# Column loads one step ahead, the u product on GpSimd, and the bonus sum ahead of the mask in a chunked linear-attention kernel

## The chip, the cores and the metric

The kernel runs on one core of one Trainium2 chip. The metric is the device time of one execution in microseconds. Three runs of the kernel before gave 383.59, 384.34 and 384.41 us, a median of 384.34 us. One further execution was profiled; it took 385.27 us, and its trace spans 383.5 us from the first instruction to the last.

## The reference

Three stages follow one another: a gated linear attention with a bonus term, a soft mixture of experts (MoE), and a feed-forward layer.

```python
# attention: B, H, S, D = 4, 8, 768, 48
for t in range(S):
    kt, vt, rt = (k[:, :, t], v[:, :, t], r[:, :, t])
    cur = np.einsum('bhd,bhe->bhde', u[None] * kt, vt)
    y[:, :, t] = np.einsum('bhd,bhde->bhe', rt, state + cur)
    state = w[None, :, :, None] * state + np.einsum('bhd,bhe->bhde', kt, vt)
# soft MoE: logits = x @ phi; softmax over tokens, 8 experts (384 x 1024 x 384) on 4 slots each,
# softmax over slots to combine
# feed-forward: h = x @ w_in; g = h * sigmoid(1.702 * h); out = g @ w_out      (384 -> 2048 -> 384)
```

## The kernel before

The attention is computed in 6 chunks of 128 tokens. A chunk has one **step** for each of the 4 batches, so there are 24 steps; this text numbers them n = 4 * chunk + batch, and calls them step 0 to step 23. Chunk 0 and chunk 5 are written out; chunks 1 to 4 are one loop body of four steps that each engine runs four times.

For each step three tensors are loaded by the SP queue: `rk` (r and k with channels on partitions, "the columns", 512 KB), `kr` (k and r with tokens on partitions, "the tokens", 384 KB) and `v` (192 KB). `rk` and `kr` are double buffered. The SP queue is in order: a load whose buffer is not free holds up every load behind it. `load_rk(n)` (L262) waits until VectorE has scaled step n - 2; `load_kr(n)` (L271) waits until GpSimd has made the scaled keys `kk` of step n - 2; behind them come `v` and a piece of the expert weights `w1` (L284).

What the engines do for step n:

- VectorE, `scale(n)` (L766): two tensor_tensor, columns times powers of w, out of a table in PSUM, into `rks`. It waits for the columns and for `rs_used`, which TensorE counts up at `earlier`.
- GpSimd, `bonus(n)` (L1199): the product k * r into `rkn`, and, from chunk 1 on, a second one, `rkn` times u (`ubc`, u on all partitions). In chunk 0 that second product is VectorE's (L782). Then `scaled_keys(n)` (L1211), then `bonus_values(n)` (L1219): v times the bonus sums, into `vd`.
- VectorE, `bonus_sum(n)` (L775): one reduction of `rkn` over the channels into `dds`; `bonus_values(n)` waits for it.
- TensorE, `scores` (L370), which waits for both masks of the step before and for `rks`; VectorE, `mask(n)` (L788): two copy_predicated that move the scores that count from PSUM to `at`.
- TensorE, in the order of its step n (L481): `logits` of the chunk before (batch 1 only), `earlier(n - 1)` (the old state's part of the output), `scores(n)`, in chunk 0 only `bonus_turns(n - 1)`, then `outputs(n - 1)`, `state(n - 1)`, small transposes (`turns` in batch 1), `tokens(n - 2)`, and from step 3 on `bonus_turns(n)`, which transposes `vd` of the same step and waits for it (`vd_ok`, L394); `gather` in batch 2.
- ScalarE: `decay` multiplies the state by w^128 (four small activations), `columns` and `rows` move results out of PSUM. `new_state(n)` (L803) on VectorE adds the chunk's part to the state.

VectorE's order inside step n before (L846): `slot_max` of the last chunk (batch 1), then `scale(n + 1)`, `mask(n)` (in steps 1 to 3 the other way round), `bonus_sum(n + 1)`, `running` of the last chunk (batch 3), `new_state(n - 1)`. The bonus sum of a step is thus taken in the step in front of it.

In chunk 5, GpSimd has extra work: after `bonus_values(21)` it makes the `own` tiles (L1245), after `bonus_values(22)` a subtraction over 128x640, and before `bonus_values(23)` a product over 128x640 (L1240), whose factor comes from VectorE's `row_sum` and that one from ScalarE's exponential of the subtraction. TensorE waits for that product (`c_ok`) in step 23.

After step 23 the MoE (to about 157 us) and the feed-forward (to the end) follow, on TensorE nearly without a gap.

Of the kernel before, what the change touches and what calls it, by code (L numbers as in the profile page):

```python
# [12 lines left out]
P = 128  # L13
# [29 lines left out]
WARM = 10  # L43
# [8 lines left out]
def rwkv_soft_moe_ffn(nc, rk, kr, v, wcol, u, phi, w1, w2, win, wout, ident, strict, match, jsel, sel, parts, out):  # L52
    with ExitStack() as ctx:
# [10 lines left out]
        def sem(name):  # L64
# [127 lines left out]
            sem(n) for n in ("lt_ps", "l_ok", "cm_ok", "nm_ok", "ex_ok", "al_ok", "tr_ps", "tr_ok", "p_ps", "run_ok"))  # L192
        nm_new, l_new, mask_go, tiles_go = (sem(n) for n in ("nm_new", "l_new", "mask_go", "tiles_go"))
# [65 lines left out]
        def _(sp):  # L259
# [28 lines left out]
            def step(c, b, first, count):  # L288
                load_rk(c, b)
                load_kr(c, b)  # L290
                load_v(c, b)
                load_w1(first, count)
# [3 lines left out]
            load_kr(0, 0)  # L296
            load_rk(0, 1)
            load_v(0, 0)
            load_kr(0, 1)
            load_v(0, 1)  # L300
            step(0, 2, 0, 0)
# [57 lines left out]
        def _(pe):  # L359
# [10 lines left out]
            def scores(c, b):  # L370
# [11 lines left out]
                if is_first(c, b):  # L382
# [4 lines left out]
                    keep_warm(LG, 7)  # L387
# [331 lines left out]
        def _(dve):  # L719
# [55 lines left out]
            def bonus_sum(c, b):  # L775
                n = B * c + b
                if is_first(c):

                    dve.wait_ge(rk_ok, n + 1)
                    if b == 0:  # L780
                        dve.wait_ge(s_const, 16 * 2)
                    dve.tensor_tensor(rkn[:, b % 2, :, :], rkn[:, b % 2, :, :], ubc[:, :, :], ALU.mult)\  # L782
                       .then_inc(rku_ok, 1)
# [4 lines left out]
            def mask(c, b):  # L788
                n = B * c + b
                if is_first(c, b):  # L790
                    dve.wait_ge(zeroed, 5)
                    dve.wait_ge(s_const, 16 * 2)
# [10 lines left out]
            def new_state(c, b):  # L803
                n = B * c + b
                dve.wait_ge(st_ps, n + 1)
                dve.wait_ge(sdec, HP * (n + 1))
# [39 lines left out]
            def step(c, b):  # L846
# [4 lines left out]
                if is_first(c) and b:  # L851
                    mask(c, b)
                    scale(*following(c, b))
                else:
                    if more:
                        scale(*following(c, b))
                    mask(c, b)
                if is_last(c) and b == 2:
                    row_sum(*early)
                if more:  # L860
                    bonus_sum(*following(c, b))
# [132 lines left out]
        def _(act):  # L994
            act.dma_start(idt[:, :], ident).then_inc(s_ident, 16)
            for dst, src in ((ubc[:, :, :].rearrange("p h e -> p (h e)"), u.partition_broadcast(P)),
                             (keep[:, :], strict)):
                act.dma_start(dst, src).then_inc(s_const, 16)
# [58 lines left out]
            def step(c, b):  # L1057
# [5 lines left out]
                if not is_first(c, b):  # L1063
                    if not is_last(prev(c, b)[0]):
# [126 lines left out]
        def _(pool):  # L1191
# [7 lines left out]
            def bonus(c, b):  # L1199
# [6 lines left out]
                if is_first(c):  # L1206
                    return
                pool.wait_ge(rk_ok, n + 1)
                pool.tensor_tensor(rkn[:, s, :, :], rkn[:, s, :, :], ubc[:, :, :], ALU.mult).then_inc(rku_ok, 1)
# [117 lines left out]
```

## Time and profile before

| | us |
|---|---|
| median of three runs | 384.34 |
| profiled execution, its own time | 385.27 |
| its span (first to last instruction) | 383.5 |
| TensorE busy in the span | 369.9 (96%) |
| VectorE / ScalarE / GpSimd busy | 235.0 / 189.4 / 94.5 |
| chunk 0 and start, up to the first TensorE instruction of chunk 1's first step | 0 to 26.1 |
| chunks 1 to 5 | 26.1 to about 119 |
| granted TensorE clock | 1.000 throughout |

Times in the trace are microseconds from the start of the span. A merged row (xN) covers N instructions that follow one another. GpSimd is POOL, VectorE is DVE, ScalarE is ACT, TensorE is PE in the rows. The bracket at a row's end says how long the engine sat idle before it and what ended the wait. The start of a matmul row is when it begins; the next one begins before the modelled end of the one before.

### The profile page before, as it was taken

The numbers are of one execution on the slowest core, as the hardware profiler recorded it, in microseconds if no ns is written. First come the engines' busy times: TensorE is split into PE (matmuls) and PEld (weight loads), VectorE is DVE, ScalarE is ACT, GpSimd is POOL, SyncE is SP. The second block draws the span as 40 slices with busy tenths as digits, with TensorE's granted clock in tenths as the row PEclk, the third lists the DMA queues.
The fourth block names the chain that finished last, engine by engine and source line by source line (L and its number), as shares of the span: only waits on it lengthen the run. The fifth ranks groups of instructions, "written<-read, shape, count | busy, mean of one in ns | idle before, by whom it ended". The sixth has DMA issues, their size and how long they took to land.

```text
span 383.5 us, 9099 instructions
## 1 busy us (share of the span) xinstructions
PE 369.9 (96%) x3206; PEld 290.6 (76%) x3206; DVE 235.0 (61%) x433; ACT 189.4 (49%) x409; POOL 94.5 (25%) x110
## 2 busy tenths in 40 slices
PE   5698999999999999999999999999999999999996
PEld 5677788878777344577888888888888888888885
DVE  6978787878774301587756556555555555555550
ACT  1344554545434440676564456445644564465452
POOL 4678788878682020100000000000000000000000
PEclk9999999999999999999999999999999999999999
DMA  7899999999999999600011002000200020002002
GB/s 234 286 333 344 400 393 405 399 393 354 405 327 409 390 414 413 249 0 2 1 46 38 0 0 84 0 0 0 82 0 0 0 82 0 0 0 82 0 2 82
DMA packets 21797, 63.76 MB, mean 166 GB/s; under 512 B 3088, under 2 KB 6816, under 8 KB 21392
## 3 DMA queue, kind: packets, MB, share of 16 engines
q1 hardware_dynamic: 20864, 63.09, 43.4%
q10 hardware_dynamic: 912, 0.39, 0.5%
q8 instruction: 14, 0.23, 0.2%
q14 instruction: 7, 0.06, 0.0%
HBM read 58.75 MB, written 4.72 MB: 165 GB/s over the span
## 4 chain that ended last, share of the span: by engine, by line
PE 92%; DVE 2%; DMA 2%; issue 1%; ACT 1%; POOL 1%; SPq 0%; DVEq 0%; ACTq 0%
PE bank L638 11%; PE bank L637 11%; PE bank L636 11%; PE bank L378 6%; PE pair L426 6%; PE pair L636 6%; PE pair L637 6%; PE pair L638 6%; PE bank L623 4%; PE pair L414 3%; PE pair L397 3%; PE bank L585 3%; PE bank L447 3%; PE bank L565 2%; DMA vb<-v 2%; PE bank L438 2%
## 5 line engine op out<-in xcount | busy, mean ns | idle before, releaser
L926 DVE TENSOR_TENSOR gf<-bank,sg 128x512 f32<-128x512 f32 x72 | 49.8, 691 | 58.3 <-ACT sg L1133 58.0
L1133 ACT ACTIVATE sg<-bank 128x512 f32<-128x512 f32 x72 | 42.9, 598 | 71.0 <-PE bank L623 71.0
L637 PE MATMUL bank<-ghi,whi 128*128 128x512 f32 x190 | 73.9, 389 | 0.0
L636 PE MATMUL bank<-glo,whi 128*128 128x512 f32 x190 | 73.9, 389 | 0.0
L638 PE MATMUL bank<-ghi,wlo 128*128 128x512 f32 x190 | 73.9, 389 | 0.0
L937 DVE TENSOR_TENSOR glo<-gf,ghi 128x512 fp32r<-128x512 f32 x96 | 66.3, 691 | 0.3
L1139 ACT ACTIVATE ghi<-gf 128x512 fp32r<-128x512 f32 x95 | 59.3, 624 | 1.8 <-DVE gf L926 1.7
L636 PEld LDWEIGHTS bank<-glo,whi 128*128 128x128 f32 x190 | 35.7, 188 | 7.4
L637 PEld LDWEIGHTS bank<-ghi,whi 128*128 128x128 f32 x190 | 35.7, 188 | 7.4
L638 PEld LDWEIGHTS bank<-ghi,wlo 128*128 128x128 f32 x190 | 35.7, 188 | 7.4
L772 DVE TENSOR_TENSOR rks<-rkb,bank 112x512 f32<-112x512 f32 x48 | 30.8, 681 | 15.4 <-PE pair L414 10.9
L636 PE MATMUL pair<-glo,whi 128*128 128x512 f32 x95 | 37.3, 392 | 0.0
L637 PE MATMUL pair<-ghi,whi 128*128 128x512 f32 x95 | 37.0, 389 | 0.0
L638 PE MATMUL pair<-ghi,wlo 128*128 128x512 f32 x95 | 37.0, 389 | 0.0
L798 DVE COPY_PREDICATED at<-keep,bank 128x512 f32<-128x512 int32 x48 | 32.5, 730 | 1.3 <-PE bank L378 0.9
L378 PE MATMUL bank<-rks 48*128 48x128 f32 x384 | 27.9, 284 | 5.2 <-DVE rks L772 3.9
L926 DVE TENSOR_TENSOR gf<-pair,sg 128x512 f32<-128x512 f32 x24 | 16.6, 692 | 23.8 <-ACT sg L1133 23.7
L378 PEld LDWEIGHTS bank<-rks 48*128 48x128 f32 x384 | 23.4, 187 | 9.5 <-issue 8.0
L1016 ACT ACTIVATE yt<-pair 112x512 f32<-112x512 f32 x24 | 14.3, 598 | 30.0 <-PE pair L426 30.0
L623 PE MATMUL bank<-ct,mst 128*128 (+1 forms) x72 | 27.9, 392 | 0.5 <-DVE mst L964 0.4
L1204 POOL TENSOR_TENSOR rkn<-krb 128x384 f32<-128x384 f32 x24 | 24.1, 1004 | 12.2 <-DMA krb<-kr 11.9
L426 PE MATMUL pair<-at,vb 128*48 128x128 f32 x384 | 25.9, 277 | 0.0
(179 smaller groups left out, 512.3 us busy)
## 6 DMA issues: line engine op xcount, KB each, us to landing
ring<-w SPq DMA_DIRECT2D x24, 512.0 KB, 6.3
rkb<-rk SPq DMA_DIRECT2D x23, 512.0 KB, 6.2
krb<-kr SPq DMA_DIRECT2D x24, 384.0 KB, 5.5
ring<-w SPq DMA_DIRECT2D x4, 1536.0 KB, 14.3
ring<-w SPq DMA_DIRECT2D x8, 768.0 KB, 8.4
vb<-v SPq DMA_DIRECT2D x24, 192.0 KB, 5.5
out<-ob SPq DMA_DIRECT2D x18, 256.0 KB, 2.1
ring<-win SPq DMA_DIRECT2D x3, 1024.0 KB, 14.3
```

The source lines that it names most:

```text
L378: last = pe.matmul(SC[i][:, hp * CH:(hp + 1) * CH], rks[s, b % 2, 1, hp, :], rks[s, b % 2, 0, hp, :], start=True, stop=True)
L426: last = pe.matmul(YT[i][o0:o0 + D, a * CH:(a + 1) * CH], vb[:, b, 2 * (a + 2 * w) + i, :], at[:, b % 2, i, a + 2 * w, :], start=False, st ...
L623: pe.matmul(HB[f % 4][:, :], mst[:, f * P:(f + 1) * P], ct_flat[:, bass.ds(i * TT, TT)], start=True, stop=True).then_inc(hh_ps, 1)
L636: pe.matmul(o, w_hi, lo, start=(f == 0), stop=False)
L637: pe.matmul(o, w_hi, hi, start=False, stop=False)
L638: pe.matmul(o, w_lo, hi, start=False, stop=(f == KF - 1)).then_inc(prod_ps, 1)
L772: dve.tensor_tensor(rks[a, b % 2, x, :, :], rkb[a, b % 2, x, :, :], w[a, :, :], ALU.mult)\
L798: dve.copy_predicated(at[:, b % 2, half, :, :], keep[:, :].unsqueeze(1).to_broadcast([P, 4, CH]), SC[half][:, :].rearrange("p (h t) -> p h ...
L926: dve.tensor_tensor(gf[:, f % 2, :], bank[f % 4][:, :], sg[:, f % 2, :], ALU.mult).then_inc(gf_ok, 1)
L937: dve.tensor_tensor(glo[:, f % 4, :], gf[:, f % 2, :], ghi[:, f % 4, :], ALU.subtract)\
L1133: act.activation(sg[:, f % 2, :], bank[f % 4][:, :], ACT.Sigmoid, scale=1.702).then_inc(sg_ok, 1)
L1139: act.activation(ghi[:, f % 4, :], gf[:, f % 2, :], ACT.Copy).then_inc(ghi_ok, 1)
```

## The change

- The SP queue asks for the columns of step n + 1 before the tokens of step n. Inside each step the order of issues is `rk(n + 1)`, `kr(n)`, `v(n)`, `w1`. The start keeps its order and asks for `rk(2)` at its end.
- u is loaded in the SP queue behind the first tokens, no more in ScalarE's queue; it has a semaphore of its own.
- In chunk 0, too, GpSimd multiplies by u.
- VectorE's step n has one order for all chunks: `scale(n + 1)`, `bonus_sum(n)`, `mask(n)`. `bonus_sum(0)` is still taken ahead of step 0.
- The decays of the state in steps 0, 1 and 2 are left out (the state is still zero there), and `new_state` waits for one less chunk of them.
- One matmul less in each of the two blocks that keep TensorE busy at the start.

```diff
-WARM = 10
+WARM = 9
@@ SP
             def step(c, b, first, count):
-                load_rk(c, b)
+                if not (is_last(c) and b == B - 1):
+                    load_rk(*following(c, b))
                 load_kr(c, b)
                 load_v(c, b)
                 load_w1(first, count)
@@
             load_rk(0, 0)
             load_kr(0, 0)
+            sp.dma_start(ubc[:, :, :].rearrange("p h e -> p (h e)"), u.partition_broadcast(P)).then_inc(s_u, 16)
             load_rk(0, 1)
             load_v(0, 0)
             load_kr(0, 1)
             load_v(0, 1)
+            load_rk(0, 2)
             step(0, 2, 0, 0)
             step(0, 3, 0, 0)
@@ TensorE, scores(0, 0)
-                    keep_warm(LG, 7)
+                    keep_warm(LG, 6)
@@ VectorE
             def bonus_sum(c, b):
                 n = B * c + b
-                if is_first(c):
-                    dve.wait_ge(rk_ok, n + 1)
-                    if b == 0:
-                        dve.wait_ge(s_const, 16 * 2)
-                    dve.tensor_tensor(rkn[:, b % 2, :, :], rkn[:, b % 2, :, :], ubc[:, :, :], ALU.mult)\
-                       .then_inc(rku_ok, 1)
                 dve.wait_ge(rku_ok, n + 1)
@@ mask
-                    dve.wait_ge(s_const, 16 * 2)
+                    dve.wait_ge(s_const, 16)
@@ new_state
-                dve.wait_ge(sdec, HP * (n + 1))
+                if is_first(c):
+                    dve.wait_ge(s_new, 1)
+                else:
+                    dve.wait_ge(sdec, HP * (n - B + 2))
@@ step
-                if is_first(c) and b:
-                    mask(c, b)
+                if more:
                     scale(*following(c, b))
-                else:
-                    if more:
-                        scale(*following(c, b))
-                    mask(c, b)
+                if not is_first(c, b):
+                    bonus_sum(c, b)
+                mask(c, b)
                 if is_last(c) and b == 2:
                     row_sum(*early)
-                if more:
-                    bonus_sum(*following(c, b))
@@ ScalarE
-            for dst, src in ((ubc[:, :, :].rearrange("p h e -> p (h e)"), u.partition_broadcast(P)),
-                             (keep[:, :], strict)):
-                act.dma_start(dst, src).then_inc(s_const, 16)
+            act.dma_start(keep[:, :], strict).then_inc(s_const, 16)
@@
-                    if not is_last(prev(c, b)[0]):
+                    if not is_first(prev(c, b)[0]) and not is_last(prev(c, b)[0]):
                         decay(*prev(c, b))
@@ GpSimd, bonus
-                if is_first(c):
-                    return
                 pool.wait_ge(rk_ok, n + 1)
+                if is_first(c, b):
+                    pool.wait_ge(s_u, 16)
                 pool.tensor_tensor(rkn[:, s, :, :], rkn[:, s, :, :], ubc[:, :, :], ALU.mult).then_inc(rku_ok, 1)
```

## Rows read from the trace of the kernel before

**Rows 1.** The page, the chain that ended last, shares of the span by engine.
```profile
PE 92%; DVE 2%; DMA 2%; issue 1%; ACT 1%; POOL 1%; SPq 0%; DVEq 0%; ACTq 0%
```
**Rows 2.** Busy time by stretch: chunk 4, all engines in turn, clock, DMA share, GB/s.
```profile
83.00:101.00 18.00, 18.00 (x329) 14.95 (x330) 14.55 (x29) 9.09 (x30) 14.08 (x15) 1.00 0.99 373
```
**Rows 3.** TensorE's timeline, steps 4 and 5: start, length, engine, line, tiles.
```profile
26.10 0.65 PE L414 MATMUL pair<-rks,st 48*48 48x128 f32 x16
...
33.05 0.42 PE L414 MATMUL pair<-rks,st 48*48 48x128 f32 x4 [1.20 <-issue]
```
**Rows 4.** VectorE's timeline in chunk 0.
```profile
9.13 0.56 DVE L782 TENSOR_TENSOR rkn<-rkn,ubc 128x384 f32<-128x384 f32 x1 [0.47 <-POOL rkn L1204]
...
13.14 1.34 DVE L782 TENSOR_TENSOR rkn<-rkn,ubc 128x384 f32<-128x384 f32 x1 [0.42 <-POOL rkn L1204]
14.51 0.55 DVE L786 TENSOR_REDUCE dds<-rkn 128x8 f32<-128x384 f32 x1
14.98 1.34 DVE L798 COPY_PREDICATED at<-keep,bank 128x512 f32<-128x512 int32 x2
```
**Rows 5.** GpSimd's timeline in chunks 0 and 1.
```profile
8.10 1.00 POOL L1204 TENSOR_TENSOR rkn<-krb 128x384 f32<-128x384 f32 x1 [3.98 <-DMA krb<-kr]
10.35 0.83 POOL L1226 TENSOR_TENSOR vd<-vb,dds 128x384 f32<-128x384 f32 x1 [1.26 <-DVE dds L786]
11.14 1.00 POOL L1216 TENSOR_TENSOR kk<-krb,wkn 128x384 f32<-128x384 f32 x1
12.10 1.00 POOL L1204 TENSOR_TENSOR rkn<-krb 128x384 f32<-128x384 f32 x1
...
24.93 1.01 POOL L1209 TENSOR_TENSOR rkn<-rkn,ubc 128x384 f32<-128x384 f32 x1
```
**Rows 6.** DMA issues and busy time by stretch, at the start.
```profile
ubc<-u ACTq DMA_DIRECT2D x1, 192.0 KB, 5.7
...
4.00:6.00 2.00, 2.00 (x12) 2.00 (x11) 1.19 (x12) 0.00 (x0) 0.12 (x1) 1.00 0.78 173
```
**Rows 7.** TensorE's timeline: end of chunk 3, start of chunk 4.
```profile
78.76 0.65 PE L414 MATMUL pair<-rks,st 48*48 48x128 f32 x16
...
82.96 0.65 PE L414 MATMUL pair<-rks,st 48*48 48x128 f32 x16
...
86.48 0.65 PE L397 MATMUL pair<-idt,vd 128*112 128x128 f32 x4
```
**Rows 8.** VectorE's timeline beside them.
```profile
79.55 1.29 DVE L772 TENSOR_TENSOR rks<-rkb,bank 112x512 f32<-112x512 f32 x2 [1.63 <-PE pair L414]
...
82.46 0.14 DVE L837 COPY stat<-stat 128x1 f32<-128x1 f32 x1
...
83.80 0.35 DVE L807 TENSOR_TENSOR st<-st,bank 112x192 f32<-112x192 f32 x1 [0.29 <-DVE acc L840]
84.39 1.28 DVE L772 TENSOR_TENSOR rks<-rkb,bank 112x512 f32<-112x512 f32 x2 [0.23 <-issue]
```
**Rows 9.** Chunk 5: TensorE's, GpSimd's and VectorE's timelines.
```profile
113.84 0.65 PE L397 MATMUL pair<-idt,vd 128*112 128x128 f32 x4 [0.17 <-ACT yt L1016]
...
118.77 0.60 PE L397 MATMUL pair<-idt,vd 128*112 128x128 f32 x4
...
106.11 0.18 POOL L1245 MEMSET own<- 128x96 f32 x1
...
107.61 1.01 POOL L1204 TENSOR_TENSOR rkn<-krb 128x384 f32<-128x384 f32 x1
...
111.16 1.26 POOL L1251 TENSOR_TENSOR lnat<-lnat,rm 128x640 f32<-128x640 f32 x1
...
107.17 1.28 DVE L772 TENSOR_TENSOR rks<-rkb,bank 112x512 f32<-112x512 f32 x2 [0.20 <-PE pair L414]
...
114.44 0.82 DVE L821 TENSOR_REDUCE rm<-lnat 128x20 f32<-128x640 f32 x1 [0.41 <-ACT lnat L1055]
```
**Rows 10.** The tile krb: from issue to landing.
```profile
DMA to landing us min/median/max: 3.2/5.5/8.4
```

More of the change, by code:

```diff
@@ L192, in rwkv_soft_moe_ffn @@
             sem(n) for n in ("lt_ps", "l_ok", "cm_ok", "nm_ok", "ex_ok", "al_ok", "tr_ps", "tr_ok", "p_ps", "run_ok"))
+        s_u = sem("s_u")
         nm_new, l_new, mask_go, tiles_go = (sem(n) for n in ("nm_new", "l_new", "mask_go", "tiles_go"))
```

## Prediction

> **What bounds the kernel now.** I read the chain of waits first, then the busy time by stretch, then the timelines of the engines side by side. The chain runs over TensorE for 92% of the span [rows 1]. In chunk 4 TensorE is busy 18.00 of 18.00 us, GpSimd 14.08, VectorE 14.55, and the DMA engines have a share of 0.99 at 373 GB/s [rows 2]. So from chunk 1 on TensorE sets the pace, and two other things stand close behind it: the DMA engines, and any result that TensorE needs just in time. Only the first 26.10 us are different. There TensorE waits again and again for VectorE and GpSimd, until `earlier(3)` opens the steps of chunk 1 at 26.10 [rows 3]. One further gap stands in step 5: 1.20 us before 33.05, which no semaphore ends ("issue") [rows 3].
>
> From this follow two rules for the sum. What is saved before 26.1 moves all that comes later forward, one for one. And from then on any wait put into TensorE's order costs its full length, as nothing behind it is idle.
>
> I write T(n) for the time at which `earlier(n - 1)` starts on TensorE in step n.
>
> **The start (a gain).** Before, VectorE multiplies by u itself: 0.56 us when GpSimd is at rest, 1.34 us beside GpSimd's product at 13.14, then the sum 0.55 and two masks 1.34 [rows 4]. After, the product by u is GpSimd's and costs 1.01 there [rows 5].
>
> The first tokens land at about 8.10 [rows 5]. u is 192 KB, took 5.7 us to land and shared the engines with the first columns and tokens, at 173 GB/s in the stretch 4:6 [rows 6]. Queued behind the tokens it no longer delays them: 192 KB are 0.5 us at the chunk rate and 1.1 us at 173 GB/s, and nothing if the rate at the start is set otherwise. I take 0.7. Then k * r of step 0 runs 7.4 to 8.4, the u product 8.5 to 9.5 (u has landed by then), the sum 9.5 to 10.05. Call its end D = 10.05 (before: 9.13 + 0.56 + 0.55, about 10.25 [rows 4]).
>
> From D on GpSimd is the chain of chunk 0. Its pitches are `vd` 0.79 (10.35 to 11.14) and 0.96 (11.14 to 12.10) for a product of 1.00 [rows 5]; the u product waits 0.1 for the one before it. One batch is therefore 0.79 + 0.96 + 0.96 + 1.06, about 3.8. The u products end at D + 3.9, D + 7.8 and D + 11.6, and each releases a sum (0.55), the masks (1.25) and the next scores. After the last one come `kk` 0.96 and `vd` 0.85, so `bonus_turns(3)` can start at D + 13.45 = 23.5. I add 0.3 for the tokens of step 2, now behind the columns of step 3 in the queue, and 0.55 for the turns themselves: T(4) = 24.3 against 26.10, a gain of **1.8**. The bounds are 0.65 (tokens no earlier, the tokens of step 2 late by 0.75) and 2.6 (tokens earlier by 1.2, no wait behind them). VectorE's masks end earlier than that chain at each batch, so they are covered.
>
> A rule of the Trainium skill speaks against this part: "GPSIMD Engine Reference", section 4.1, says to put elementwise products on VectorE, as GpSimd takes about twice the time. The rows agree on the ratio (1.01 against 0.56), but the product that ran beside GpSimd took 1.34 [rows 4], and section 8 of the same page names the reason, shared SBUF interfaces. By the rule alone the four moves would cost 4 x 0.45 = 1.8 us, and chunk 0 would gain nothing. What decides is the order, as the sum is now off the masks' way; so I do not follow it.
>
> No cost: the two dropped warm-up matmuls lie in TensorE's idle time ahead of the scores (the granted clock is 1.00 throughout [rows 2, 6]); the dropped decays lie on ScalarE, which waits most of the time; they come back nowhere, since the state is zero. The mask's u wait was long over.
>
> The 1.20 us gap in step 5 stays in my sum. It is at one place of the code, in the first pass through the loop. The Trainium skill, "Runtime: NRT & Kernel Launch", section "Instruction fetch mechanics", says instructions come in blocks by DMA; no row shows that this gap is such a fetch.
>
> **The tokens behind the columns (a small loss).** Before, `kr(n)` is asked for when `kk(n - 2)` is done. After, it stands behind `rk(n + 1)`, which waits for the scaling of step n - 1, that is until T(n - 2) + 0.79 + 1.3 [rows 7, 8]; with the issue of the columns, about T(n - 2) + 2.8. It must land by T(n) - 0.4, as k * r, times u, `kk` and `vd` (3.9 us) follow on GpSimd before TensorE wants `vd`. Two steps last 9.1 to 9.3 us, so 5.9 us are left, against a median to landing of 5.5, a least of 3.2 and a most of 8.4 [rows 10]. Hence between 0 and 2.5 us in a step. With the DMA engines full [rows 2], 512 KB more ahead of it are 1.3 us later in the queue; in chunk 0 the engines gain about that back. I take **0.3** for the whole, while the lead is largest (chunks 1 and 2).
>
> **The bonus sum one step later (the main loss).** Before, the sum of step n was taken in step n - 1, a whole step ahead of its use. After, it stands behind `scale(n + 1)`, which cannot start before T(n) + 0.79 (79.55 - 78.76) [rows 7, 8]. Then: two scalings 1.20, sum 0.55, `vd` 0.08 + 0.83, TensorE's start 0.05. So `bonus_turns(n)` can start at T(n) + 3.50. TensorE gets there at T(n) + 3.52 (86.48 - 82.96) [rows 7]. In an ordinary step the cover is just gone and costs nothing; for missed hundredths over some fifteen steps I add **0.2**, bounds 0 and 1.5 (0.1 each).
>
> In the first step of a chunk it is not enough. There VectorE comes late out of step n - 1, where it has `running` of the last chunk (82.46 on) and `new_state` (83.80): its scaling starts at 84.39, T(16) + 1.43 [rows 7, 8]. The new order of step 15 holds the same instructions, so this time stays. Then the sum starts at 85.59, ends 86.14, `vd` ends 87.05, and TensorE starts 87.1 where it started 86.48: **0.6** late. That holds for the first steps of chunks 2, 3 and 4: 1.8 us. In chunk 5, out of the loop, VectorE is quicker; I take 0.2. Bounds for one step: 0.3 (if `running` moves up) and 0.8.
>
> In chunk 5 GpSimd's extra work stands between. Before, `own` (106.11 to 107.61, 1.50 us) came with a step in hand [rows 9]. After: `scale(22)` starts at 107.17 as before [rows 9], sum of step 21 to 108.9, `vd` to 109.8, `own` to 111.3, k * r and u of step 22 (2.1) to 113.4, sum to 114.0, `vd` to 114.9; TensorE's turns of step 22 start at 114.95, before at 113.84 [rows 9]: 1.1 late. Next on GpSimd the subtraction, 1.26 [rows 9], to 116.15; ScalarE's exponential of as many columns (0.8, taken as long as VectorE's pass over them [rows 9]) and VectorE's row sum with its two small ones (1.3) give the factor at 118.3; GpSimd has made the products of step 23 by then; the product over 128x640 to 119.6, `vd(23)` to 120.45. TensorE turns it at 120.5, before at 118.77 [rows 9]: **1.7** late in all, the 1.1 included. Bounds 1.0 and 2.5.
>
> **The sum.** -1.8 + 0.3 + 0.2 + 1.8 + 0.2 + 1.7 = +2.4 us. From the end of chunk 5 on TensorE's chain passes this on. The profiled execution took 385.27 us (span 383.5 and 1.8 around it), so a like execution would take 387.7; the median of the runs lies 0.93 lower, and the forecast against it is 384.34 + 2.4 = **386.7 us**.
>
> **The rivals.**
>
> (a) *The late sum does not hold TensorE up* (faster). Place: `bonus_turns(n)` in the first steps of chunks and in chunk 5. If `vd` were there when TensorE arrives, only the start counts: 384.34 - 1.8 + 0.3 = 382.8. It decides at 0.6 us of slack per first step. For it: VectorE is busy only 14.55 of 18.00 us [rows 2], so it could run ahead. Against it: it cannot, since scaling waits for `earlier` on TensorE (idle 1.63 us for it [rows 8]). Chance 0.22.
>
> (b) *The tokens become the bound.* If the latency stays at 6.8 us, between the median and the most, against 5.9, steps lose 0.9; in four of the eight steps of chunks 1 and 2 that is 3.6 in place of 0.3: 390.0. For it: the DMA share of 0.99. Against it: loads asked for in one burst find a shorter queue. Chance 0.10.
>
> (c) *The 1.20 us gap of step 5 goes with the shifted traffic.* If it is a fetch held up by the DMA queue, as the page on the runtime would have it, a queue less full removes it: 385.5. Chance 0.12.
>
> (d) *The start gains nothing*, because the first tokens are no earlier and u lands late behind them: 388.5. Chance 0.05.
>
> My forecast has 0.51.
>
> **How the numbers follow.** A measurement of this kernel can tell about 0.2% (0.77 us) from no change. Slower by more: 0.47 of the forecast's 0.51, 0.10 of (b), 0.08 of (c), 0.05 of (d), none of (a), 0.70. Within: 0.03, 0.03 of (c) and 0.05 of (a), 0.11. Faster: 0.01, 0.01 and 0.17, 0.19. The forecast's own range is 385.3 to 388.2. As (a) holds most of the rest I reach down to 382.9 and up to 389.0.
>
> **What would show it.** Right: `earlier(3)` near 24.3; u products at 1.0 on GpSimd in chunk 0; TensorE's turns waiting for GpSimd's `vd` in the first steps of chunks 2 to 4, 0.6 us each, and T(n) + 3.5 elsewhere; chunk 5 with waits of about 1.1 for `vd(22)` and 0.6 more in step 23. The turns of step 23 stand near 121.2 (118.77 + 2.4). Wrong: no wait at the turns (rival a); GpSimd idle for `krb` before late turns (b); no gap in step 5 (c); T(4) near 26 (d).

## The result: 389.4 us, 1.2% slower than before

| | median | runs | ratio to before (95%) |
|---|---|---|---|
| before | 384.38 us | 383.59 to 384.62 | 1 |
| changed kernel | 389.40 us | 388.43 to 390.32 | 1.0115 [1.0086, 1.0144] |

The ratios here and below leave out executions that were over 1.5% longer than the fastest of the same kernel, which are one of e6 and one of e9.

The profiled execution took 389.44 us (span 387.6) against 385.27 (span 383.5): 4.1 us between the two traces, 5.0 between the medians. (The profiled execution of the kernel before is its longest; its other four took 383.59 to 384.62.) The forecast was a loss of 2.4 us and 386.7, so the direction was right and the loss was about twice the size forecast. The median lies 0.4 us above the upper end of the stated range, 389.0; taken by the ratio, 384.34 * 1.0115 = 388.8, it lies inside. All of the 4.1 us is there by the end of the attention: the turns of step 23 start at 122.85, before at 118.77, that is 4.08 later.

The page of the changed kernel, the chain that ended last, by engine. It answers [rows 1], where TensorE had 92%:

```profile
PE 79%; DMA 7%; POOL 5%; DVE 3%; issue 3%; SPq 1%; ACT 0%; DVEq 0%; POOLq 0%; ACTq 0%
```

The largest part of the new chain that is not TensorE is the load of the tokens, `krb<-kr`, with 6% of the span by the page's list by line. Busy time by stretch, columns as in [rows 2]: the start, and chunk 4.

```profile
14.00:16.00 2.00, 2.00 (x19) 1.77 (x19) 2.00 (x4) 0.00 (x0) 2.00 (x3) 0.59 1.03 385
16.00:18.00 2.00, 2.00 (x30) 1.91 (x28) 1.14 (x4) 0.60 (x1) 1.80 (x3) 0.56 0.86 337
87.00:105.00 18.00, 17.25 (x308) 14.17 (x310) 13.50 (x29) 8.37 (x28) 13.99 (x15) 1.00 0.96 357
```

In chunk 4 TensorE is busy 17.25 of 18.00 us where it was never idle; at 14 to 18 its granted clock is 0.59 and 0.56, so mostly the lower level of 1.2 GHz. Chunk 0 on GpSimd and VectorE, answering [rows 4, 5] (timelines: start, length, engine, line, tiles, idle time before and what ended it):

```profile
6.12 1.00 POOL L1200 TENSOR_TENSOR rkn<-krb 128x384 f32<-128x384 f32 x1 [2.00 <-DMA krb<-kr]
8.68 1.01 POOL L1205 TENSOR_TENSOR rkn<-rkn,ubc 128x384 f32<-128x384 f32 x1 [1.56 <-DMA ubc<-u]
10.45 0.83 POOL L1222 TENSOR_TENSOR vd<-vb,dds 128x384 f32<-128x384 f32 x1 [0.77 <-DVE dds L784]
...
9.72 0.55 DVE L784 TENSOR_REDUCE dds<-rkn 128x8 f32<-128x384 f32 x1 [2.63 <-POOL rkn L1205]
```

The tokens are there 2.0 us earlier, and most of that time (1.56 us idle) is spent waiting for u, which now lands last. The first sum starts at 9.72; before it could start at 9.13 + 0.56 = 9.69 [rows 4]. TensorE's timeline, answering [rows 3]:

```profile
12.77 1.16 PE L383 MATMUL bank<-rks 48*128 48x128 f32 x16 [2.51 <-DVE at L796]
...
14.48 1.95 PE L431 MATMUL pair<-at,vb 128*48 128x128 f32 x16
...
24.95 0.65 PE L419 MATMUL pair<-rks,st 48*48 48x128 f32 x16
...
30.20 0.65 PE L419 MATMUL pair<-rks,st 48*48 48x128 f32 x16
```

T(4) is 24.95 in place of 26.10, and the gap of 1.20 us inside `earlier(4)` is gone. TensorE stood idle 2.51 us before the scores of step 1, and the outputs after them took 1.95 us at the lower clock, where those of later steps take 1.08.

The first step of chunk 4 is step 16. The issues of SyncE (the engine that issues the SP queue's loads, SPq in the rows), GpSimd, VectorE and TensorE, answering [rows 7, 8]:

```profile
73.38 0.93 SPq L287 DMA_DIRECT2D ring<-w  x2
75.89 0.33 SPq L270 DMA_DIRECT2D rkb<-rk  x1
76.48 0.34 SPq L278 DMA_DIRECT2D krb<-kr  x1
...
83.87 1.00 POOL L1200 TENSOR_TENSOR rkn<-krb 128x384 f32<-128x384 f32 x1 [1.92 <-DMA krb<-kr]
...
86.86 0.84 POOL L1222 TENSOR_TENSOR vd<-vb,dds 128x384 f32<-128x384 f32 x1
...
83.87 1.29 DVE L777 TENSOR_TENSOR rks<-rkb,bank 112x512 f32<-112x512 f32 x2 [0.23 <-issue]
86.07 0.55 DVE L784 TENSOR_REDUCE dds<-rkn 128x8 f32<-128x384 f32 x1 [0.91 <-POOL rkn L1205]
...
82.69 0.65 PE L419 MATMUL pair<-rks,st 48*48 48x128 f32 x16
...
87.75 0.65 PE L402 MATMUL pair<-idt,vd 128*112 128x128 f32 x4 [1.41 <-POOL vd L1222]
```

The columns are asked for at 75.89, as soon as VectorE has scaled step 15's; the tokens of step 16 come 0.59 us behind them and land 7.2 us later, at T(16) + 1.2. GpSimd idles 1.92 us for them, VectorE's sum waits 0.91 for GpSimd, and TensorE waits 1.41 for `vd`. The chain of waits (start, length, what) goes the same way:

```profile
75.01 0.69 DVE rks L777
75.89 0.33 SPq L270
76.48 7.23 DMA krb<-kr
83.88 1.00 POOL rkn L1200
84.95 1.00 POOL rkn L1205
```

Chunk 5, GpSimd's timeline, then VectorE's sum of step 22, then TensorE's turns of steps 22 and 23, answering [rows 9]:

```profile
112.58 0.30 POOL L1242 TENSOR_TENSOR own<-same,jcol 128x64 fp32r<-128x64 f32 x1
113.39 1.00 POOL L1200 TENSOR_TENSOR rkn<-krb 128x384 f32<-128x384 f32 x1 [0.51 <-DMA krb<-kr]
...
116.14 0.83 POOL L1222 TENSOR_TENSOR vd<-vb,dds 128x384 f32<-128x384 f32 x1 [0.66 <-DVE dds L784]
...
120.65 1.27 POOL L1236 TENSOR_TENSOR lnat<-lnat,rm 128x640 f32<-128x640 f32 x1 [0.42 <-DVE rm L827]
121.87 0.83 POOL L1222 TENSOR_TENSOR vd<-vb,dds 128x384 f32<-128x384 f32 x1
...
115.50 0.55 DVE L784 TENSOR_REDUCE dds<-rkn 128x8 f32<-128x384 f32 x1 [1.30 <-POOL rkn L1205]
...
117.11 0.62 PE L402 MATMUL pair<-idt,vd 128*112 128x128 f32 x4 [1.73 <-POOL vd L1222]
122.85 0.62 PE L402 MATMUL pair<-idt,vd 128*112 128x128 f32 x4 [0.16 <-POOL vd L1222]
```

One table holds the account. For each step it has the time from T(n) to the start of `bonus_turns(n)`, read off TensorE's timeline; e4 and e5 are experiments told below.

| step | before | changed | e4 | e5 |
|---|---|---|---|---|
| 4 | 3.53 | 3.66 | 3.66 | 3.66 |
| 5 | 5.31 | 3.91 | 4.73 | 3.99 |
| 8 | 3.53 | 4.00 | 4.47 | 4.45 |
| 9 | 3.71 | 4.00 | 4.00 | 3.98 |
| 12 | 3.53 | 4.80 | 4.11 | 4.57 |
| 16 | 3.52 | 5.06 | 4.50 | 4.49 |
| 20 | 3.49 | 3.79 | 4.23 | 4.24 |
| 21 | 3.45 | 3.63 | 3.63 | 3.64 |
| 22 | 3.46 | 5.02 | 4.47 | 4.46 |
| 23 | 3.57 | 4.41 | 4.41 | 4.41 |

A difference can be larger than the wait for `vd` in the row, as it holds all idle time of TensorE between the two points. All other steps of the changed kernel stand within 0.01 us of before. Changed less before: T(4) -1.15; step 4 +0.13; step 5 -1.40; first steps 8, 12 and 16 +0.47, +1.27, +1.54, together +3.28; step 9 +0.29; chunk 5 +0.30, +0.18, +1.56, +0.84, together +2.88. The sum is +4.03, of 4.08 measured.

### The profile page after: what moved, and what is told of

Its sections match the earlier page's. It is cut to its first block, busy times and chain, and to the rows that moved or that the text cites. A ratio compares the mean times of both kernels' runs of the same rounds, so it can differ in the third digit from the quotient of the medians.

```text
span 387.6 us, 9076 instructions
## 1 busy us (share of the span) xinstructions
PE 372.3 (96%) x3202; PEld 291.9 (75%) x3202; DVE 231.1 (60%) x429; ACT 186.3 (48%) x397; POOL 98.4 (25%) x114
## 4 chain that ended last, share of the span: by engine, by line
PE 79%; DMA 7%; POOL 5%; DVE 3%; issue 3%; SPq 1%; ACT 0%; DVEq 0%; POOLq 0%; ACTq 0%
PE bank L641 11%; PE bank L643 11%; PE bank L642 11%; DMA krb<-kr 6%; PE pair L641 6%; PE pair L642 6%; PE pair L643 6%; PE bank L628 4%; PE pair L431 3%; PE bank L590 3%; PE bank L383 3%; PE bank L570 2%; PE pair L402 2%; DMA vb<-v 2%; PE pair L419 2%
## 5 line engine op out<-in xcount | busy, mean ns | idle before, releaser
L924 DVE TENSOR_TENSOR gf<-bank,sg 128x512 f32<-128x512 f32 x72 | 49.7, 691 | 58.3 <-ACT sg L1129 58.0
L431 PE MATMUL pair<-at,vb 128*48 128x128 f32 x384 | 26.8, 283 | 0.0
```

The costliest lines, as they stand in the source:

```text
L431: last = pe.matmul(YT[i][o0:o0 + D, a * CH:(a + 1) * CH], vb[:, b, 2 * (a + 2 * w) + i, :], at[:, b % 2, i, a + 2 * w, :], start=False, st ...
L924: dve.tensor_tensor(gf[:, f % 2, :], bank[f % 4][:, :], sg[:, f % 2, :], ALU.mult).then_inc(gf_ok, 1)
```

## The experiments

The theory (A) was: TensorE, which works in order, waits in the first steps of the chunks and in chunk 5 for the late `vd`. Two causes of the lateness could be told apart: the tokens land too late (A2), or VectorE and GpSimd come too late by their own order (A3). The rivals were that the load order alone is the cause (B), that the early start is given back anyway (C), and that VectorE and GpSimd are the bound and TensorE's wait only shows it (D). Ratios are to the kernel before on the same chip (medians 385.15, 385.01 and 384.98 us over 17 to 23 runs).

**The changed kernel once more.** No edit. 

> The changed kernel once more, unchanged, as the reference for the runs beside it on the same chip: 1.011 of the kernel before (1.0086 to 1.0144 measured).

Measured: 391.78 us (389.81 to 394.11), ratio 1.0174 [1.0135, 1.0213], above the 1.011 expected. These six executions lie 4.3 us apart, the 17 of the kernel before beside them 2.6. The profiled one took 392.66 us, and its turns of step 23 start at 126.04, 3.2 us later than in the first trace. Three rows show most of it (the scores of step 1 on TensorE, then the tokens and the turns of step 11):

```profile
12.74 2.08 PE L383 MATMUL bank<-rks 48*128 48x128 f32 x16 [3.00 <-DVE at L796]
...
61.95 1.01 POOL L1200 TENSOR_TENSOR rkn<-krb 128x384 f32<-128x384 f32 x1 [2.12 <-DMA krb<-kr]
...
65.84 0.65 PE L402 MATMUL pair<-idt,vd 128*112 128x128 f32 x4 [0.94 <-POOL vd L1222]
```

T(4) is 26.41 in place of 24.95: up to the scores of step 1 nothing differs by more than 0.1 us on VectorE and GpSimd, but TensorE then runs at the lower clock from those scores on (granted clock 0.64, 0.50, 0.50 and 0.65 in the four stretches from 12 to 20, where the first trace has 1.00, 0.59, 0.56 and 1.00). So in this execution the start gained nothing; it lost 0.3 us. In step 5 TensorE waits 1.10 us for VectorE's scaling (4.87 in the table's terms, against 3.91). Step 11, an ordinary step, stands at 4.58, since its tokens land late. Steps 8, 9, 20 and 21 are as in the first trace, steps 12 and 16 stand at 4.86 and 5.25, step 22 at 4.46, step 23 at 4.41. The waits in the first steps and in chunk 5 keep their place, though not their size; what comes on top moves from execution to execution.

**e1: only the sum back to its early place.**

```
-                if more:
+                if is_first(c) and b:
+                    mask(c, b)
                     scale(*following(c, b))
-                if not is_first(c, b):
-                    bonus_sum(c, b)
-                mask(c, b)
+                else:
+                    if more:
+                        scale(*following(c, b))
+                    mask(c, b)
...
+                if more:
+                    bonus_sum(*following(c, b))
```

> The changed kernel, but the bonus sum of step n + 1 is again taken in step n behind the mask, as before; the loads keep the new order (columns of n + 1 ahead of tokens of n). Theory A (the late sum put 5 waits of TensorE for vd on its path, about 6 us; the load order is only what makes some of them longer): the waits for vd at the turns go. But now the tokens of step n + 1, asked for late, must be there one step earlier, so VectorE waits for GpSimd's product in most steps, by 2 to 3 us, and the scaling behind it starts about 1 us later than at T + 0.8. That is still in time for most scores: 384 to 388 us. Theory B (the load order alone is the cause, the sum's place is free): no better than the changed kernel, 389 or more.

Measured: 404.87 us (403.25 to 407.81), ratio 1.0524 [1.0490, 1.0559]. That is far above theory A's 384 to 388; theory B had set no upper end (389 or more), and e2 decides against it. Its waits up to 125 us, and SyncE's up to 130 (us in total, times, longest):

```profile
POOL rkn L1204 <- DMA krb<-kr: 35.6, 21, 2.9
DVE dds L784 <- POOL rkn L1209: 34.1, 20, 3.4
...
SPq L270 <- DVE rks L777: 61.3, 21, 5.4
```

This is a ring. VectorE's sum of step n + 1, taken in step n, needs the tokens n + 1; they stand in SyncE's order behind the columns n + 2, which wait for VectorE's scaling of step n; and the next scaling stands behind that sum. In the chain of this run: scaling from 64.76, tokens asked for at 66.23, landed after 5.72, two products to 74.20.

**e2: only the loads back to their old order.**

```
             def step(c, b, first, count):
-                if not (is_last(c) and b == B - 1):
-                    load_rk(*following(c, b))
+                load_rk(c, b)
```

(and the load of step 2's columns ahead of the steps goes.) 

> The changed kernel, but the loads of each step in the order of before (columns n, tokens n, v, w1). The bonus sum stays late. Theory A: each first step of chunks 2 to 4 still loses 0.6 us at the turns (VectorE comes late from the step in front), and chunk 5 still loses 2 to 2.5; only the extra 1.0 and 1.3 us of chunks 3 and 4, where the tokens landed late, go: 387 to 387.8. Theory B: back to before or better, 382 to 384.5.

Measured: 398.09 us (395.25 to 400.55), ratio 1.0328 [1.0291, 1.0366]. Both theories (A: 387 to 387.8, B: 382 to 384.5) missed it. Its waits up to 125 us, and SyncE's:

```profile
DVE rks L774 <- DMA rkb<-rk: 14.7, 9, 3.3
PE pair L399 <- POOL vd L1219: 10.6, 11, 2.1
...
SPq L278 <- POOL kk L1209: 49.7, 20, 5.2
```

With the sum late, GpSimd's `vd(n)` is late, and `kk(n + 1)` behind it. The tokens wait for `kk` on SyncE (49.7 us over 20 issues; in the kernel before 27.3 over 18), and under the old order the columns stand behind the tokens, so VectorE's scaling waits for columns. The new order lets them out first.

**e3: both back.** Only the start of the change stays: u in the inputs' queue, GpSimd's product by u in chunk 0, the shorter warm-up and the left-out decays. 

> Both undone: bonus sum early and loads in the old order; what stays is u in the SP queue behind the first tokens, GpSimd's product by u in chunk 0, the dropped decays and the two dropped warm-up matmuls. Theory A: no wait at the turns, TensorE keeps its lead of the start (1.2 us, 2.4 if the 1.2 us gap of step 5 also stays away): 382 to 383.3. Rival C (the lead of the start is given back anyway, as the DMA engines are full in chunks 1 to 4): 384.4, as before. If the gap of step 5 is back, it hangs on the load order or the sum's place and not on u.

Measured: 384.58 us (383.65 to 385.85), ratio 0.9987 [0.9976, 0.9998], span 383.1. No turn waits for `vd`; all steps from 4 on stand within 0.1 us of before. So the loss belongs to the pair, late sum and new load order: by the ratios the late sum costs 13 us with the old loads (1.0328 less 0.9987), the new loads cost 21 us with the early sum (1.0524 less 0.9987), and together they cost 5 (1.0115 less 0.9987). The load order is a repair that the late sum needs. And the start, alone, is worth about 0.1%.

**e7: u between the first columns and the tokens.** e3 with two lines exchanged. 

> The version with early sum and old load order, with u loaded between the first columns and the first tokens. In the changed kernel u landed at 8.65, 2.5 us after the tokens at 6.1 although it is only 192 KB, and GpSimd's product by u waited 1.6 us for it. If u's slow load is what eats the gain of the start: u lands by 6.5 to 7, tokens by 7 to 7.5, the sum of step 0 ends 0.6 to 1.0 earlier (9.3 to 9.7), TensorE's idle time ahead of step 1 falls below 2 us and its clock stays at 2.4 GHz, T(4) 24.3 to 25.0 against 25.55: 0.4 to 1.2 us faster than without it (0.9987 of before), so 0.9955 to 0.998. Rival: columns and tokens are delayed by u's whole transfer and nothing is won: 0.9985 or more.

```
             load_rk(0, 0)
+            sp.dma_start(ubc, u).then_inc(s_u, 16)
             load_kr(0, 0)
-            sp.dma_start(ubc, u).then_inc(s_u, 16)
```

Measured: 385.36 us (384.76 to 386.55), ratio 1.0011 [0.9996, 1.0026]. u lands after 5.5 us in place of 6.4, but GpSimd's k * r starts at 8.26 and the product by u at 9.33. T(4) is 26.11, as before the change. The last of the three loads lands a little earlier than in e3 (GpSimd's first use of it starts at 8.26, in e3 at 8.69), but now it is the tokens, and two products stand behind them where one stands behind u.

**e8: more warm-up.** e3 with `keep_warm(LG, 14)` in place of 6. 

> The version with early sum and old load order (0.9987 of before), with 14 instead of 6 warm-up matmuls behind the first scores. There TensorE is idle for 2.7 us ahead of the scores of step 1 and its granted clock then falls to 0.5 in the stretch 14:16. If the idle time is what costs the clock: clock 1.0 in chunk 0, outputs and state of step 1 in 1.6 instead of 2.8 us, T(4) at 25.0 to 25.3 against 25.55, ratio 0.997 to 0.9985. Rival: chunk 0 is bound by GpSimd anyway and the slow clock is hidden: T(4) 25.5, ratio 0.9987 or above.

Measured: 384.44 us (383.72 to 385.59), ratio 0.9989 [0.9977, 1.0000]. The stretch 14 to 16 in e3 and then in e8 (columns as above):

```profile
14.00:16.00 2.00, 2.00 (x16) 1.64 (x18) 1.65 (x3) 0.00 (x0) 2.00 (x3) 0.50 1.02 336
```
```profile
14.00:16.00 2.00, 1.34 (x32) 1.22 (x32) 2.00 (x4) 0.60 (x1) 2.00 (x3) 1.00 0.98 343
```

The granted clock is 1.00 in place of 0.50, TensorE has 32 instructions in 1.34 us where it had 16 in 2.00, and T(4) is 24.98 in place of 25.55: 0.57 us. The runs don't show it: 0.9987 and 0.9989 are one ratio.

**e10: u alone.** The kernel before with u in SyncE's queue, all else as it was. 

> The kernel before with one edit: u is loaded in the SP queue behind the first tokens, nothing else is changed (VectorE still multiplies by u in chunk 0). Columns and tokens of step 0 land 1.6 and 2 us earlier as in the changed kernel, u 1.7 us later than before. VectorE's product then waits for u until 8.65, it took place at 9.13 before: the start gains 0.4 to 0.5, T(4) 25.5 to 25.8: ratio 0.9985 to 0.9995. Rival: the gain of the version with both undone came from GpSimd's product by u, so nothing here: 1.000.

```
             load_rk(0, 0)
             load_kr(0, 0)
+            sp.dma_start(ubc, u).then_inc(s_u, 16)
             load_rk(0, 1)
```

Measured: 384.84 us (383.97 to 386.09), ratio 0.9993 [0.9974, 1.0012]. T(4) is 25.58, but the clock is at the lower level here too (0.50 in 14 to 16, after 1.71 us idle). No change to be told in the runs. Its trace, like those of e7 and e8, has the early sum and no idle time marked as issue in step 5, and all three lose time in steps 8 and 9 all the same: step 8 stands at 4.16 (e10), 4.10 (e7) and 4.43 (e8), step 9 at 3.90, 3.90 and 3.91. In step 8 TensorE waits there for `new_state`, which VectorE reaches late:

```profile
47.23 0.56 PE L440 MATMUL bank<-vb,kk 128*48 128x48 f32 x16 [0.44 <-DVE st L809]
```

**e4: the double piece of w1 in the second step of a chunk, not in the fourth.**

```
-    ((B + 1) * (c - 1) + b, 1 if b < B - 1 else 2)
+    ((B + 1) * (c - 1) + b + (1 if b > 1 else 0), 2 if b == 1 else 1)
```

> The changed kernel, but of the five pieces of w1 in each chunk the doubled one is loaded in the second step and not in the fourth. Theory A2 (the tokens of a chunk's first step land 7 us after their issue since they stand behind two pieces of w1 and the next columns): in the first steps of chunks 3 and 4 the wait at the turns falls from 1.15 and 1.4 us in the rows to 0.4 as in chunk 2, so 387.4 to 388.2; the tokens of the third step are late instead, where VectorE is early and 0.5 us of it are covered. Rival: the latency comes from elsewhere (the DMA engines full in general), waits unchanged, 389.4.

Measured: 390.92 us (389.81 to 392.55), ratio 1.0163 [1.0142, 1.0183]: no gain. The table shows the reason: steps 12 and 16 fell by 0.69 and 0.56 us, as was expected with 512 KB less ahead of their tokens, but steps 8 and 20 rose by 0.47 and 0.44, and step 5 by 0.82. Step 22 fell by 0.55.

**e5: w1 behind the attention.** All loads of w1 are moved behind the last step, and the experts' part waits 14.0 us for them, so only the time up to the turns of step 23 is read.

```
                 load_v(c, b)
-                load_w1(first, count)
...
+            load_w1(0, KD * E)
             load_w2(0)
```

> The changed kernel, but all 24 pieces of w1 are loaded behind the last tokens and values of the attention, in the same queue; the MoE then waits for them, so the whole time is of no use (some 15 to 30 us more) and only the stretch up to the turns of step 23 is read. Theory A2 (in the first steps of chunks 3 and 4 and in step 22 the tokens land too late since w1 fills the queue ahead of them; VectorE's lateness is only 0.5 of it): without w1 the tokens land in 3.5 to 4.5 us, the turns of the first steps of chunks 2 to 4 wait 0.3 to 0.5 us in the rows each and no more, step 22 waits 1.1 (own tiles), and the turns of step 23 stand at 120 to 120.7 against 122.85. Rival A3 (all of the wait is VectorE and GpSimd order, the landing is beside it): turns of step 23 as in the changed kernel, 122.5 to 123.2.

Measured: 414.96 us (one run); the turns of step 23 start at 124.00, no earlier than with w1 there (122.85). The start was 0.79 us later in this trace (T(4) 25.74); counted from T(4) it is 98.26 us against 97.90. GpSimd never waits for tokens in the loop. Yet steps 8, 12 and 16 stand at 4.45 to 4.57 and step 22 at 4.46. VectorE and then TensorE around step 8 in e5, and below it VectorE in the changed kernel:

```profile
44.20 0.68 DVE L840 SCALAR_TENSOR_TENSOR stat<-stat 128x1 f32<-128x1 f32 x1
...
46.31 1.28 DVE L777 TENSOR_TENSOR rks<-rkb,bank 112x512 f32<-112x512 f32 x2 [0.25 <-issue]
...
49.17 0.65 PE L402 MATMUL pair<-idt,vd 128*112 128x128 f32 x4 [0.80 <-POOL vd L1222]
```
```profile
43.29 0.21 DVE L840 SCALAR_TENSOR_TENSOR stat<-stat 128x1 f32<-128x1 f32 x1
...
44.93 1.28 DVE L777 TENSOR_TENSOR rks<-rkb,bank 112x512 f32<-112x512 f32 x2 [0.25 <-issue]
```

The scaling of step 9, ahead of the sum of step 8, starts at T(8) + 1.59 in e5 and at T(8) + 1.15 in the changed kernel. A2's 120 to 120.7 was missed, and A3's 122.5 to 123.2 is met only without those 0.79 us; nor are the tokens beside the matter, as steps 12 and 16 fell by 0.23 and 0.57. A better account follows: two paths end in `vd`, VectorE's (running, new state, scaling, sum) and the tokens' (load, two products, sum), and the later one decides. VectorE's path gives 4.00 where GpSimd is idle beside it (step 8 of the changed kernel) and 4.45 to 4.57 where it isn't (e5), 0.47 to 1.04 over the 3.53; the tokens' path, where they are late, gives up to 5.06 (5.25 in the second trace). Taking w1 away only exchanged the one for the other. For step 8 this is not the whole: kernels with the early sum stand at 4.10 to 4.43 there too, when step 5 has no gap (see e10).

**e6: the sum ahead of the scaling in the first steps of chunks.**

```
+                if b == 0 and not is_first(c, b):
+                    bonus_sum(c, b)
                 if more:
                     scale(*following(c, b))
-                if not is_first(c, b):
+                if b:
                     bonus_sum(c, b)
```

> The changed kernel, but in the first step of every chunk (not of chunk 0) the bonus sum is taken ahead of the scaling, in the other steps behind it. VectorE's part of the wait (scaling 1.2 us ahead of the sum) is taken away there. Theory A2: chunk 2's first step loses its 0.4 us, in chunks 3 and 4 the wait stays above 0.8, as it hangs on tokens that land at T + 1; the sum then also holds the scaling up. In all 0 to 0.7 us faster than the changed kernel. Theory A as I predicted it (VectorE's lateness is the whole of it): all first steps lose their waits, 3 us faster, 386.5 or less on the first chip's scale.

Measured: 391.17 us (388.19 to 394.08), ratio 1.0147 [1.0111, 1.0184], beside 1.0174 for the changed kernel on the same chip: no gain that can be told. In its trace tokens decide again, since a sum put first waits for them first: VectorE idles 3.13 us for step 8's product and TensorE 2.10 for its `vd`. The edit is not shown to be the cause, as e9, which has no such edit, waits 2.12 us at the same place, with its tokens just as late. (The profiled executions of e6 and e9 were the longest of their kernels, 394.08 and 393.33 us, so sizes from these two traces are to be taken with care.)

**e9: the own tiles a step earlier.** `own` after step 20 in place of step 21 (`b == 0` for `b == 1`). 

> The changed kernel, but GpSimd makes the own tiles of chunk 5 behind the values of step 20 and not of step 21. My step in the prediction: own (1.5 us) between the values of step 21 and the product of step 22 costs 1.1 at the turns of step 22. Then the turns of step 22 come at T + 3.5 to 3.9 instead of T + 4.5 to 5.0, and 1 us is won in all. Rival (tokens of step 22 land late, 0.5 us of idle GpSimd in the changed kernel's rows): T + 4.5, 0.3 us won or nothing.

Measured: 389.39 us (387.04 to 393.33), ratio 1.0106 [1.0079, 1.0134]. The turns of step 22 stand at 3.88 (4.46 to 5.02 with `own` behind step 21), while step 20 rose to 4.22 from 3.79:

```profile
120.96 0.62 PE L402 MATMUL pair<-idt,vd 128*112 128x128 f32 x4 [0.59 <-POOL vd L1222]
```

TensorE still waits 0.59 us there, in place of 1.17 to 1.73. So `own` is the cause of 0.6 to 1.1 us of the wait at step 22, and not of all of it. The rise in step 20 is not `own`'s doing, which stands behind `vd(20)`: GpSimd idled 1.15 us for the tokens there. What the move is worth in all lies within the changed kernel's scatter.

**e11: the turns later on TensorE.** If the in-order wait is the loss, it must shrink when TensorE does something else first. In a chunk's first step the turns go behind `logits`, in its third behind `gather`.

```
                     logits(c - 1)
+                    bonus_turns(c, 0)
...
-                if not is_first(c) or b == B - 1:
-                    bonus_turns(c, b)
                 if tail and b == 2:
                     gather(c - 1, LG, 2 * c)
+                if b and (not is_first(c) or b == B - 1):
+                    bonus_turns(c, b)
```

> The changed kernel, but TensorE does other ready work ahead of the turns that wait: in the first step of a chunk the turns stand behind the logits of the next step (1.0 us), in the third behind the gather (0.8 us). VectorE, GpSimd and the queue do the same. Theory A (the loss is TensorE's wait in order for vd, and nothing else): the first steps of chunks 2 to 5 win back up to 1.0 us each, 0.3 + 1.0 + 1.0 + 0.3, and step 22 0.8, some 3 us in all; ratio 1.002 to 1.007 where the changed kernel has 1.0115 and 1.0174. Rival D (GpSimd and VectorE are the bound and TensorE's wait only shows it): the wait comes back in the next steps, ratio 1.011 or more.

Measured: 387.77 us (386.05 to 389.01), ratio 1.0068 [1.0043, 1.0092]. TensorE's turns in steps 12 and 13, then in step 16, and what is left in step 22:

```profile
68.08 0.65 PE L402 MATMUL pair<-idt,vd 128*112 128x128 f32 x4
72.71 0.65 PE L402 MATMUL pair<-idt,vd 128*112 128x128 f32 x4 [0.18 <-POOL vd L1223]
...
86.96 0.65 PE L402 MATMUL pair<-idt,vd 128*112 128x128 f32 x4
...
115.37 0.62 PE L402 MATMUL pair<-idt,vd 128*112 128x128 f32 x4 [1.12 <-POOL vd L1223]
```

No first step waits any more, though the tokens are late here too (GpSimd idles 1.16, 1.21, 1.07 and 1.52 us for them in steps 8, 12, 16 and 20). `vd` of these four steps is ready at T(n) + 4.27, 4.35, 4.21 and 4.46, in the changed kernel at 3.95, 4.75, 5.01 and 3.64: other sizes, but the same in sum. The turns of step 23 start at 121.11, 1.74 us earlier than in the changed kernel. Theory A holds: with `vd` as late on the whole and another thing to do first, TensorE loses less. The time itself bears it out less sharply than the trace: the interval of e11 reaches up to 1.0092, that of the changed kernel's first runs down to 1.0086. What stays are waits of 0.40 us in step 9 and 0.18 in step 13, and chunk 5. No version that keeps the late sum came back to the time of before.

## Why the forecast had the sign and half the size

**The start: -1.15 measured, -1.8 forecast.** The first sum ends at 10.27 (D was to be 10.05) because u lands last, 0.2 us of the miss. Most of the rest is TensorE's clock, as far as e3 against e8 goes: idle for 2.51 us, it then ran at the lower level, and in e8, where more warm-up kept it at the higher one, the start is 0.57 us shorter. In the second trace of the changed kernel the lower level came sooner and lasted longer, and the start lost 0.3 us. The prediction used the granted clock of before (1.00 [rows 2, 6]) to call the dropped warm-up free; that step failed, as the earlier columns put TensorE's first work earlier and its idle time after it grew from 1.30 to 2.51. Rival (d) was nearer to the truth in the runs than in the trace: alone, the start gave 0.13% [0.02, 0.24] (e3), about 0.5 us.

**The gap in step 5: -1.40, forecast 0.** Rival (c) came true in the profiled execution, but e4 has 0.95 us of such idle time again, e9 0.71, e11 0.50 (there ahead of the scores), and e10, with only u moved, has none. The second trace of the changed kernel waits 1.10 us at the same place, there for VectorE's scaling. The gap is tied to none of the edits tried, and what it is stays open. Nor is all of the 1.40 kept: the early-sum kernels without the gap (e7, e8, e10) lose 0.76 to 1.10 us in steps 8 and 9, and the two that lose as much in step 5 as before (before itself, by the gap, and e3, by other waits) lose nothing there. Without this gain the loss in the trace would have been 5.5 us (4.1 + 1.4), which is nearer to the 5.0 between the medians.

**Ordinary steps: right in the profiled execution.** T(n) + 3.53 in 10, 11, 14, 15, 18 and 19, where `vd` was worked out for T(n) + 3.50. The cover is just gone, and 0.2 us for missed hundredths were not needed. Step 9 lost 0.29. In the second trace late tokens cost 1.05 us in step 11, which is rival (b)'s mechanism in an ordinary step.

**First steps of chunks 2 to 4: +3.28 measured, 1.8 (with the tokens 2.1) forecast.** This is the step that was mis-sized. The mechanism, `vd` held up behind scaling and sum, was right, and the wait stood where it was put. In step 8, with 0.47 of the 3.28, the late sum may not be the cause, as e7, e8 and e10, with the early sum and no gap in step 5, lose as much there; steps 12 and 16, with 2.81 us, lose nothing in any of the three. But the prediction added the two causes up separately: 0.6 from VectorE, and for the tokens 0.3 for the whole, held to fall in chunks 1 and 2 while the lead is largest. The tokens' load took 6.92 us for step 12 and 7.23 for step 16, against the 5.9 left to it and the median of 5.5 [rows 10] (5.7 after); rival (b) had used 6.8 for four steps and priced the lot at 390.0, which the runs came near to, in part by luck, since the gap of step 5 and the size of chunk 5 are no part of it. (A slip by the way: 512 KB at 373 GB/s are 1.4 us, not 1.3; no term hangs on it.) And the price of a late token is not taken off a reserve, as the sum no longer has one. VectorE's path alone costs 0.47 to 1.04 (step 8, and e5) in place of 0.6: a small operation of it takes longer when GpSimd works beside it (0.68 against 0.21 us). The term that was wrong in size is thus above all that of the tokens, 0.3 us for the whole: where they decide, steps 12 and 16 stand at 4.80 and 5.06, where 3.52 and the forecast's 0.6 give 4.1.

**Chunk 5: +2.88 measured, +1.9 forecast.** Step 22 was to be 1.1 late and is 1.56 (GpSimd idles 0.51 for tokens behind `own`, after a load of 8.08 us, then VectorE); step 23 adds 0.84 for 0.6; step 20 0.30 for 0.2; step 21 had no term and has 0.18. e9 shows `own` to be the cause of 0.6 to 1.1 us in step 22.

**Rival (a)**, that the late sum does not hold TensorE, was wrong: scaling cannot run ahead of `earlier`, as the prediction said against it.

Forecast and measured stand side by side so: start 0.65 less, step 5 1.40 more gained, first steps with tokens 1.2 more lost, chunk 5 1.0 more, steps 4 and 9 0.4 more, ordinary steps 0.2 less. That is 2.4 + 0.65 - 1.40 + 1.18 + 0.98 + 0.42 - 0.20 = 4.03, with 4.08 in the trace. So the sum is as near as it is by luck in one place: the unforeseen gain in step 5 hides 1.4 us of the misses.

## What to carry to other kernels

When a result is taken one step later, work out for each path that feeds it when it ends, and take the later one for each kind of step; a median latency does not do where the reserve is gone. A queue that issues in order ties loads to the order of their users: change either alone only after you have followed the ring from the buffer's release through the queue to the user that releases the next one. And where an engine waits in order for something just late, other work of its own put in front of the wait takes part of it back (e11: ratio 1.0068, where the changed kernel has 1.0115 and 1.0174).

## What the runs showed of the hardware

- **The order of loads and the order of users.** Four kernels differ only in these two: 384.6 us (both old), 389.4 and 391.8 (both new), 398.1 (late sum, old loads), 404.9 (early sum, new loads). The Trainium skill, "DMA: Bandwidth & Descriptors", section "Anatomy of one DMA — SWDGE (gpsimd) path", says that the wait for a semaphore happens on the issuing engine and the DMA engines only consume their queues. The trace agrees: SyncE stood 61.3 us at the columns' issue in e1 with the tokens behind it.
- **Small operations beside GpSimd.** The same 128x1 `scalar_tensor_tensor` on VectorE, with its inputs in SBUF, took 0.21 to 0.22 us in all four chunks of the changed kernel's loop, with GpSimd idle for nearly all of it, and 0.66 to 0.68 us in all four of e5, with a GpSimd operation running beside it. "GPSIMD Engine Reference" of the Trainium skill, section 8, names the SBUF interfaces that the two engines share, for VectorE instructions with two SBUF inputs among others; the trace agrees, with 0.47 us for this one instruction.
- **The clock at the start.** TensorE's idle time before step 1's scores, and the granted clock in 14 to 16: 0.69 us (e8), 1.30 (before), 1.65 (e4) and 1.73 (e5), all 1.00; 1.71 (e10) 0.50, 2.00 (e9) 0.50, 2.31 (e11) 0.55, 2.51 (changed) 0.59, 2.70 (e3) 0.50, 2.99 (e7) 0.50, 3.00 (second trace of the changed kernel) 0.50. After the long idle times it ran mostly at 1.2 GHz, after the short ones at 2.4; 1.71 and 1.73 us lie on either side, so the length of this idle time does not decide it alone. The price was 0.57 us between e3 and e8. Between the two traces of the changed kernel, which differ in when and for how long the clock was low, it was 1.46 us of T(4).
- **Scatter.** The changed kernel's runs lie 1.9 and 4.3 us apart (4 and 6 runs), those of before beside the latter 2.6 (17 runs). Its two traces differ by 3.2 us at the turns of step 23, and the parts are these: 1.5 us of the start, by the clock; 1.0 in step 5; 1.1 in step 11, where tokens landed late; 0.25 in steps 12 and 16; and 0.6 less in step 22. So late loads are one part of the scatter and the clock at the start is another; two traces don't tell how often each comes.
